# A Strassen scheme with seven block products for the first matrix of a second MLP, over pairs of token tiles

## The chip, the cores and the metric

One core of a Trainium2 chip. The time is the device time of one execution in microseconds; the kernel before takes 1283.23 us (median of 3 runs, 1282.59 to 1283.57). The engines are TensorE (PE, its weight loads PEld), VectorE (DVE), ScalarE (ACT), GpSimd (POOL), and SyncE (SP), whose queue issues nearly all DMAs.

## The reference

A linear attention over 8 batches of 8 heads, 576 tokens of 64 elements, then two MLPs over the 4608 tokens of width 512. In NumPy terms:

```python
x = attention(q, k, v).transpose(0, 2, 1, 3).reshape(4608, 512)
h = x @ w_in                                   # first network, 512 x 2048
x = (maximum(h, 0) + alpha * minimum(h, 0)) @ w_out
h = x @ w_in2                                  # second network, 512 x 1024
e = exp(h - max(h)); sm = e / (sum(e) + 1e-9)
solu = h * sm
ln = (solu - mean(solu)) / sqrt(var(solu) + 1e-6) * g_ln
out = ln @ w_out2                              # 1024 x 512
```

The change concerns `h = x @ w_in2` alone. All is float32.

## The kernel before

Every float32 operand of a large product is split in a high part (a rounded copy, written by ScalarE) and a low part (the operand less its high part, by VectorE or GpSimd), both in the type fp32r. A product is three matmuls: high by high, high by low weights, low by high weights. A matmul has a 128x128 stationary and a 128x512 moving operand.

The first network takes nine chunks of 512 tokens. For each it loops over 16 blocks `f` of the hidden width: `up(c, f)` (12 matmuls into `ps_h`), `prelu` on VectorE, `g_high` on ScalarE, `g_low` on GpSimd, and two blocks later `down(c, f)` (12 matmuls into `ps_y`). The attention of the next batch is worked in between. The result goes transposed to `y_scratch` in DRAM.

The second network takes 36 tiles of 128 tokens, written `tiles(m)` with `r` in 0 to 3. For each tile:

- SP loads `x2`; ScalarE makes `x2h` (line 769), GpSimd `x2l` (line 543).
- TensorE: `m1_product` (from line 1251), 24 matmuls with x stationary and `W2` moving, into two banks of `ps_m` or `ps_h`.
- VectorE: the negated maximum out of PSUM (line 1044). ScalarE: the exponential with its sum (line 734). VectorE: sum + eps, reciprocal, and `solu` = h * 1/sum * e, which reads h in PSUM (line 1057), its mean (line 1060). ScalarE: the squares (line 741). VectorE: variance (line 1066); GpSimd: to the power -1/2 (line 577); VectorE: `z` (line 1072) and its transpose in 32x32 blocks into `zb` (line 1078).
- SP stores `zb` to `z_scratch` (line 417) and loads it back with the blocks moved to their places as `zt`, in four DMAs (line 423). This completes the transpose. ScalarE makes `zh` (line 753), VectorE `zl` (line 1082).
- TensorE: `m2_product` (lines 1338 to 1340), 24 matmuls. ScalarE copies the result to `ost` (line 763), SP stores it.

The very last tile is transposed by TensorE instead (`z_transpose`, line 1325), since nothing is left to hide the way through DRAM.

All queues are written by hand, with counting semaphores. The order of the second network is a software pipeline: TensorE does `m1_product` of tile i + 1, then `m2_product` of tile i - 2. The first two `m1_product`s stand in the last chunk of the first network, between the last `down`s. The second network's weights are split during that chunk (lines 792 and 1035 for `w_in2`, 776 and 1024 for `w_out2`).

Of the kernel before, what the change touches and what calls it, by code (L numbers as in the profile page):

```python
# [26 lines left out]
def linear_attention_two_mlps(nc, q, k, v, w_in, w_out, alpha, w_in2, w_out2, g_ln, out):  # L27
# [24 lines left out]
    with ExitStack() as ctx:  # L52
# [7 lines left out]
        with ExitStack() as phase:  # L60
# [5 lines left out]
            qTh = sb("qTh", [P, 2, TOK], F32R)  # L66
            qTl = sb("qTl", [P, 2, TOK], F32R)
# [13 lines left out]
            kvh = sb("kvh", [P, KT, P], F32R)  # L81
            kvl = sb("kvl", [P, KT, P], F32R)
# [13 lines left out]
            mhalf = sb("mhalf", [P, 1])  # L96

# [5 lines left out]
        with ExitStack() as phase:  # L103
            W2 = sb("W2", [P, 2, KT, F2], F32R)
            WO2 = sb("WO2", [P, NF2, 2, DM], F32R)
            e2 = sb("e2", [P, 2, F2])
            solu = sb("solu", [P, 2, F2])
# [4 lines left out]
            ost = sb("ost", [P, 2, DM])  # L112
            st = sb("st", [P, 2, 10])
            zb = sb("zb", [P, F2])
            zt = sb("zt", [P, 2, F2])
# [6 lines left out]
        hbank = (ps_m, ps_h)  # L122
# [66 lines left out]
        x2_in = [sem(f"x2_in{i}") for i in range(4)]  # L189
        x2h_ok = sem("x2h_ok")  # L190
        x2l_ok = sem("x2l_ok")
        m1_done = sem("m1_done")
# [10 lines left out]
        zb_st = sem("zb_st")  # L203
        zb_ok = sem("zb_ok")
        zt_in = sem("zt_in")
# [8 lines left out]
        w2_at = {12: (0,), 13: (1, 2), 14: (3, 4), 15: (5, 6)}  # L214
        raw2 = (V[:, :, :, :].rearrange("p t h d -> p (t h d)")[:, 0:MAIN], A[:, 0:MAIN])

        x2 = (kmax[:, :].rearrange("p (a n) -> p a n", a=KT), x2b[:, :, :],
              V[:, :, :, :].rearrange("p t h d -> p (t h d)")[:, MAIN:MAIN + DM].rearrange("p (a n) -> p a n", a=KT),
              A[:, MAIN:MAIN + DM].rearrange("p (a n) -> p a n", a=KT))
        x2h, x2l = (t[:, :, :].rearrange("p s (a n) -> p s a n", a=KT) for t in (qTh, qTl))  # L220
# [8 lines left out]
        zb_out = zb[:, :].rearrange("p (j f a) -> p j f a", j=4, a=32)  # L229
# [4 lines left out]
        def z_source(r, by_pe):  # L234
            if by_pe:
                return z_blocks(ps_y[:, 0:2, :].rearrange("p a n -> p (a n)"))
# [61 lines left out]
        def _(sp):  # L298
# [93 lines left out]
            def load_x2(m, r, first=False):  # L392
                if first:
                    sp.wait_ge(y_st, 64 * (NC - 1))
                else:
                    sp.wait_ge(x2h_ok, 4 * m + r - 3)
                    sp.wait_ge(x2l_ok, 4 * m + r - 3)
                sp.dma_start(x2[r],
                             y_dram[m, :, :, r * P:(r + 1) * P].rearrange("a p n -> p a n")).then_inc(x2_in[r], 16)
# [13 lines left out]


            def store_z(m, r):
                sp.wait_ge(zb_ok, 4 * m + r + 1)
                sp.dma_start(z_dram[r % 2], zb[:, :]).then_inc(zb_st, 16)

            def load_z(m, r):

                sp.wait_ge(zb_st, 16 * (4 * m + r + 1))
                for j in range(4):
                    sp.dma_start(zt[32 * j:32 * (j + 1), r % 2, :].rearrange("b (i c) -> b i c", i=4),
                                 z_dram[r % 2].rearrange("(i b) (j c) -> j b i c", i=4, j=4)[j]).then_inc(zt_in, 16)

# [10 lines left out]
            for r in range(4):  # L436
                load_x2(0, r, first=True)
            sp.wait_ge(w2_hi, 2)
            sp.wait_ge(w2_lo, 2)
            sp.dma_start(raw2[0].rearrange("p (a n) -> p a n", a=half), w2o[:, 0:half, :]).then_inc(w2v_in, 16)  # L440
            sp.wait_ge(w2_hi, 4)
            sp.wait_ge(w2_lo, 4)
            sp.dma_start(raw2[1].rearrange("p (a n) -> p a n", a=half), w2o[:, half:NF2, :]).then_inc(w2a_in, 16)


            for r in range(4):
                if r >= 1:
                    load_z(0, r - 1)
                if r == 1:
                    store_y(LAST)  # L450
                load_x2(1, r)
                if r == 3:
                    store_out(0, 0)
                store_z(0, r)
            sp.wait_ge(y_st, 64 * NC)
            with sp.Fori(1, LAST) as m:
                for r in range(4):
                    if r == 0:
# [919 lines left out]
```

## Time and profile before

| | |
|---|---|
| median of 3 runs | 1283.23 us (1282.59 to 1283.57) |
| profiled execution | 1283.55 us, its span 1281.7 us |
| TensorE busy | 1269.4 us, 99% of the span |
| VectorE busy | 692.6 us, 54% |
| ScalarE busy | 387.3 us, 30% |
| GpSimd busy | 347.3 us, 27% |
| granted TensorE clock | 1.0 |

Busy is the time in which an engine has an instruction in execution. A matmul's row shows 0.39 us because the end of its way through the array is counted; matmuls overlap, and their pace is the distance from start to start. In the timeline the columns are start, duration, engine (SPq: a DMA issue on SP's queue), line, operation, output and inputs, and in square brackets the idle time ahead and what ended it.

### The profile page before, as it was taken

What the parts mean: (1) busy time and instruction counts of PE and PEld (TensorE: products, weight loads), DVE (VectorE), ACT (ScalarE), POOL (GpSimd) and SP (SyncE); (2) the same over time, 40 slices, a digit from 0 to 9 for tenths busy, and PEclk for the clock granted to TensorE, in tenths of its full rate; (3) what the DMA queues carried; (4) which work ended last, traced back from release to release, by engine and by line L of the source; (5) the groups of instructions that cost most, each with busy time, mean ns of one, the idle gap of its engine ahead of it and who ended that gap; (6) DMA issues with size and microseconds to landing.
All of it is one profiled execution on the core that took longest, in us unless ns stands there. A gap on an engine that the chain in (4) does not pass through costs nothing.

```text
span 1281.7 us, 16928 instructions
## 1 busy us (share of the span) xinstructions
PE 1269.4 (99%) x6277; PEld 1046.2 (82%) x6277; DVE 692.6 (54%) x965; ACT 387.3 (30%) x625; POOL 347.3 (27%) x289
## 2 busy tenths in 40 slices
PE   7999999999999999999999999999999999999998
PEld 6788888888888888888888888888888888888887
DVE  7865744644744644644644323346655555555553
ACT  4333212212222222222222212123544444444432
POOL 5333233233233234234234222222211111111110
PEclk9999999999999999999999999999999999999999
DMA  8543311311311311311310101210654444444432
GB/s 205 141 120 81 89 37 51 93 37 44 100 37 41 103 37 41 103 37 41 103 37 4 66 1 38 94 59 32 197 164 140 140 146 147 145 141 147 147 123 75
DMA packets 136017, 114.82 MB, mean 90 GB/s; under 512 B 56856, under 2 KB 117808, under 8 KB 135088
## 3 DMA queue, kind: packets, MB, share of 16 engines
q1 hardware_dynamic: 135936, 114.37, 30.2%
q8 instruction: 20, 0.33, 0.1%
q14 instruction: 13, 0.11, 0.0%
q10 hardware_dynamic: 48, 0.01, 0.0%
HBM read 76.03 MB, written 38.32 MB: 89 GB/s over the span
## 4 chain that ended last, share of the span: by engine, by line
PE 98%; DVE 1%; DMA 0%; issue 0%; POOL 0%; ACT 0%; DVEq 0%
PE ps_h L1202 10%; PE ps_y L1220 10%; PE ps_y L1218 10%; PE ps_y L1219 10%; PE ps_h L1204 10%; PE ps_h L1203 10%; PE ps_y L1339 5%; PE ps_y L1338 5%; PE ps_y L1340 5%; PE ps_h L1269 3%; PE ps_m L1273 3%; PE ps_m L1269 3%; PE ps_h L1273 3%; PE ps_m L1268 3%; PE ps_h L1268 3%; PE ps_m L1128 2%
## 5 line engine op out<-in xcount | busy, mean ns | idle before, releaser
L528 POOL TENSOR_TENSOR gl<-tg,gh 128x512 fp32r<-128x512 f32 x144 | 193.8, 1346 | 586.0 <-ACT gh L647 586.0
L647 ACT ACTIVATE gh<-tg 128x512 fp32r<-128x512 f32 x144 | 91.0, 632 | 598.4 <-PE ps_y L1220 432.3
L945 DVE TENSOR_SCALAR tg<-ps_h,acols 128x512 f32<-128x512 f32 x144 | 107.8, 748 | 242.2 <-PE ps_h L1204 240.7
L1202 PE MATMUL ps_h<-xh,W 128*128 128x512 f32 x576 | 227.5, 395 | 0.1
L1218 PE MATMUL ps_y<-gh,WO 128*128 128x512 f32 x576 | 225.3, 391 | 0.0
L1204 PE MATMUL ps_h<-xh,W 128*128 128x512 f32 x576 | 224.5, 390 | 0.0
L1220 PE MATMUL ps_y<-gh,WO 128*128 128x512 f32 x576 | 224.4, 390 | 0.0
L1203 PE MATMUL ps_h<-xl,W 128*128 128x512 f32 x576 | 224.3, 389 | 0.0
L1219 PE MATMUL ps_y<-gl,WO 128*128 128x512 f32 x576 | 224.2, 389 | 0.0
L1202 PEld LDWEIGHTS ps_h<-xh,W 128*128 128x128 f32 x576 | 108.1, 188 | 23.5 <-DVE W L936 0.5
L1204 PEld LDWEIGHTS ps_h<-xh,W 128*128 128x128 f32 x576 | 108.1, 188 | 23.0
L1220 PEld LDWEIGHTS ps_y<-gh,WO 128*128 128x128 f32 x576 | 108.1, 188 | 22.7
L1219 PEld LDWEIGHTS ps_y<-gl,WO 128*128 128x128 f32 x576 | 108.1, 188 | 22.1
L1218 PEld LDWEIGHTS ps_y<-gh,WO 128*128 128x128 f32 x576 | 108.2, 188 | 22.0
L1203 PEld LDWEIGHTS ps_h<-xl,W 128*128 128x128 f32 x576 | 108.2, 188 | 21.7
L1338 PE MATMUL ps_y<-WO,zh 128*128 128x512 f32 x288 | 112.1, 389 | 0.0
L1340 PE MATMUL ps_y<-WO,zl 128*128 128x512 f32 x288 | 112.0, 389 | 0.0
L1339 PE MATMUL ps_y<-WO,zh 128*128 128x512 f32 x288 | 112.0, 389 | 0.0
L948 DVE SCALAR_TENSOR_TENSOR tg<-ps_h,tg 128x512 f32<-128x512 f32 x144 | 99.5, 691 | 5.0
L1340 PEld LDWEIGHTS ps_y<-WO,zl 128*128 128x128 f32 x288 | 54.1, 188 | 11.3
L1338 PEld LDWEIGHTS ps_y<-WO,zh 128*128 128x128 f32 x288 | 54.0, 188 | 11.2
L1339 PEld LDWEIGHTS ps_y<-WO,zh 128*128 128x128 f32 x288 | 54.0, 187 | 11.1
(163 smaller groups left out, 1641.0 us busy)
## 6 DMA issues: line engine op xcount, KB each, us to landing
z_scratch<-zb SPq DMA_DIRECT2D x35, 512.0 KB, 2.6
zt<-z_scratch SPq DMA_DIRECT2D x140, 128.0 KB, 3.0
y_scratch<-stage SPq DMA_DIRECT2D x36, 256.0 KB, 3.1
A<-k_dram SPq DMA_DIRECT2D x16, 512.0 KB, 5.0
V<-v_dram SPq DMA_DIRECT2D x32, 256.0 KB, 4.7
out_dram<-ost SPq DMA_DIRECT2D x32, 256.0 KB, 2.3
A<-q_dram SPq DMA_DIRECT2D x14, 512.0 KB, 4.7
stage<-kx_scratch SPq DMA_DIRECT2D x6, 1024.0 KB, 4.6
```

The costliest lines, as they stand in the source:

```text
L528: nc.gpsimd.tensor_tensor(gl[:, f % 2, :], tg[:, f % 2, :], gh[:, f % 2, :].bitcast(F32), ALU.subtract).then_inc(gl_ok, 1)
L945: nc.vector.tensor_scalar(tg[:, f % 2, :], ps_h[:, f % 2, :], 0.0, slope[:, f:f + 1], ALU.min, ALU.mult).then_inc(t_ok, 1)
L948: nc.vector.scalar_tensor_tensor(tg[:, f % 2, :], ps_h[:, f % 2, :], 0.0, tg[:, f % 2, :], ALU.max, ALU.add).then_inc(g_ok, 1)
L1202: nc.tensor.matmul(o, W1[:, f, 0, a, :], xh[:, a, :], start=(a == 0), stop=False)
L1203: nc.tensor.matmul(o, W1[:, f, 0, a, :], xl[:, a, :], start=False, stop=False)
L1204: mm = nc.tensor.matmul(o, W1[:, f, 1, a, :], xh[:, a, :], start=False, stop=(a == KT - 1))
L1218: nc.tensor.matmul(o, WO[:, f, 0, cols], gh[:, f % 2, :], start=(f == 0), stop=False)
L1219: nc.tensor.matmul(o, WO[:, f, 0, cols], gl[:, f % 2, :], start=False, stop=False)
L1220: mm = nc.tensor.matmul(o, WO[:, f, 1, cols], gh[:, f % 2, :], start=False, stop=(f == NF - 1))
L1338: nc.tensor.matmul(o, zh[:, r % 2, f * P:(f + 1) * P], WO2[:, f, 0, :], start=(f == 0), stop=False)
L1339: nc.tensor.matmul(o, zh[:, r % 2, f * P:(f + 1) * P], WO2[:, f, 1, :], start=False, stop=False)
L1340: mm = nc.tensor.matmul(o, zl[:, r % 2, f * P:(f + 1) * P], WO2[:, f, 0, :], start=False, stop=(f == NF2 - 1))
```

## The change

Two tiles of 128 tokens are taken together, as a pair. x of the pair is cut in 2 x 2 blocks (two token tiles by two halves of the width 512), `w_in2` in 2 x 2 blocks of 256 x 512. Seven products of a block combination of x with one of w (Winograd's form of Strassen's scheme) give the four blocks of h:

- **Weights.** `w2_turn` on GpSimd forms the combinations in four subtractions in the last chunk; seven high parts (`w2_high`, ScalarE) and seven low parts (`w2_low`, VectorE) go to `W2c`.
- **x.** `x2_sums` on GpSimd makes four sums of 128x256 for each pair; then there are seven blocks of 128x256 to split, as one of 1024 and one of 768 elements: `x2_high` on ScalarE, `x2_low` on GpSimd (for the first two pairs VectorE). There is one buffer for these parts, free when all seven products of the pair before are done; `x2raw` has two.
- **Products.** `m1_pair` does seven groups of six matmuls in three banks (`ba`, `bb`, `bd`). The fourth adds onto the first's bank, the fifth onto the third's, the sixth onto the second's, the seventh again onto `bd`.
- **Sums out of PSUM.** ScalarE copies the first product to `p1` and the sum in `ba` to h's block 11. VectorE makes `q1`, `u1`, and the blocks c22, c12, c21 of h. h then stands in SBUF, in the tile `solu`, and the maximum, the exponential and the solu product read it there.
- **Order.** Each queue now goes pair by pair. TensorE: `m1_pair(i)`, then both `m2_product`s of pair i - 1. SP: both stores of z, then both loads. The last pair is transposed by TensorE, both tiles.
- **Start.** One `m1_pair` stands ahead of `down(14)` of the last chunk, in the place of the two single products.

TensorE's side:

```diff
+            def m1_pair(i, first=False):
+                pe.wait_ge(x2l_ok, 2 * i + 2)
+                if first:
+                    pe.wait_ge(w2_lo, 7)
+                    pe.wait_ge(g_ok, NF * LAST + 15)
+
+                def block(k, bank, more=False):
+                    a = LEFT[k] * 2 * P
+                    for j in range(2):
+                        hi, lo = (t[:, a + j * P:a + (j + 1) * P] for t in (x2h, x2l))
+                        nc.tensor.matmul(bank, hi, W2c[:, k, 0, j, :], start=(j == 0 and not more), stop=False,
+                                         skip_group_check=more)
+                        nc.tensor.matmul(bank, hi, W2c[:, k, 1, j, :], start=False, stop=False, skip_group_check=more)
+                        mm = nc.tensor.matmul(bank, lo, W2c[:, k, 0, j, :], start=False, stop=(j == 1), skip_group_check=more)
+                    mm.then_inc(prod, 1)
+
+                if not first:
+                    pe.wait_ge(c11_ok, i)
+                block(0, ba)
+                if not first:
+                    pe.wait_ge(c12_ok, i)
+                block(1, bb)
+                if not first:
+                    pe.wait_ge(c21_ok, i)
+                block(2, bd)
+                pe.wait_ge(p1_ok, i + 1)
+                block(3, ba, more=True)
+                pe.wait_ge(u1_ok, i + 1)
+                block(4, bd, more=True)
+                pe.wait_ge(q1_ok, i + 1)
+                block(5, bb, more=True)
+                pe.wait_ge(c22_ok, i + 1)
+                block(6, bd, more=True)
...
+            def pair(m, h, last=False):
+                i = 2 * m + h
+                m1_pair(i)
+                m2_product(i - 1, 0)
+                m2_product(i - 1, 1, last=(last and h == 1))
```

SP's order of a pair, its stores and loads of z:

```diff
+                for t in range(2):
+                    store_z(m, 2 * h + t)
+                if first and h == 0:
+                    sp.wait_ge(w2_lo, 7 + NF2)
+                for t in range(2):
+                    load_z(m, 2 * h + t)
```

ScalarE's:

```diff
+                p1_copy(i)
...
+                    zt_high(i - 1, 0)
+                c11_copy(i)
...
+                    zt_high(i - 1, 1)
+                if not (last and h == 1):
+                    x2_high(i + 1, 1 - h)
+                exp_tile(i, 0)
+                exp_tile(i, 1)
+                square_tile(i, 0)
+                square_tile(i, 1)
```

GpSimd's:

```diff
+            def x2_sums(i, h, m):
+                pool.wait_ge(x2_in[h], 32 * (m + 1))
+                a11, a12, a21, a22 = (x2raw[:, h, n * 2 * P:(n + 1) * 2 * P] for n in range(4))
+                s1, s2, s4 = (xsum[:, n * 2 * P:(n + 1) * 2 * P] for n in range(3))
+                if not (isinstance(i, int) and i == 0):
+                    pool.wait_ge(x2l_ok, 2 * i)
+                nc.gpsimd.tensor_tensor(s1, a21, a22, ALU.add).then_inc(xs_ok, 1)
...
+            def pair(m, h, first=False, last=False):
+                i = 2 * m + h
+                if not (last and h == 1):
+                    x2_sums(i + 1, 1 - h, m + h)
+                    if not (first and h == 0):
+                        x2_low(i + 1, 1 - h)
+                for t in range(2):
+                    power(m, 2 * h + t)
```

VectorE's order in the loop of the second network, before: two tiles (`ps_h` and `ps_m` hold h; `zl` belongs to a tile of two slots ago).

```order
L1082 TENSOR_TENSOR zl<-zt,zh 128x1024
...
L1057 SCALAR_TENSOR_TENSOR solu,st<-ps_m,st,e 128x1024
...
L1072 TENSOR_SCALAR z<-solu,st 128x1024
...
L1078 STREAM_TRANSPOSE zb<-z 128x1024
...
L1044 TENSOR_REDUCE st<-ps_h 128x1
...
L1082 TENSOR_TENSOR zl<-zt,zh 128x1024
```

And now, one pair. `kmt` is `q1`, `x2b` is `u1`, `kmax` is `p1`; the lines on `solu` with a sum are c22, c12 and c21; `A` holds what was loaded back as `zt`.

```order
L1147 TENSOR_TENSOR kmt<-ps_m,kmax 128x512
...
L1153 TENSOR_TENSOR x2b<-ps_h,kmax 128x512
...
L1162 TENSOR_TENSOR solu<-ps_h,kmt 128x512
...
L1219 TENSOR_TENSOR zl<-A,zh 128x1024
...
L1167 TENSOR_TENSOR solu<-ps_m,x2b 128x512
L1180 TENSOR_REDUCE st<-solu 128x1
...
L1171 TENSOR_TENSOR solu<-ps_h,kmax 128x512
L1180 TENSOR_REDUCE st<-solu 128x1
...
L1219 TENSOR_TENSOR zl<-A,zh 128x1024
...
L1189 SCALAR_TENSOR_TENSOR solu,st<-solu,st,e 128x1024
```

The first `zl` has moved between the sums of the pair's products, and both `zl` stand ahead of the solu products of both tiles; two normalisations with their transposes follow.

SP's queue in the same loop, before, for one tile and the start of the next:

```order
L423 DMA zt<-z_scratch 32x4x256 x4
...
L398 DMA kmax<-y_scratch 128x4x128
...
L410 DMA out_dram<-ost 128x512
...
L417 DMA z_scratch<-zb 128x1024
...
L423 DMA zt<-z_scratch 32x4x256 x4
...
L398 DMA x2b<-y_scratch 128x4x128
```

And now, for one pair (`tg` holds the output, `V` the transposed z):

```order
L435 DMA out_dram<-tg 128x512
...
L422 DMA x2raw<-y_scratch 128x4x128
...
L422 DMA x2raw<-y_scratch 128x4x128
...
L435 DMA out_dram<-tg 128x512
...
L440 DMA z_scratch<-V 128x1024
...
L440 DMA z_scratch<-V 128x1024
...
L446 DMA A<-z_scratch 32x4x256 x8
```

The load of a tile stood ahead of the next tile's store; now both stores stand ahead of both loads.

## Rows read from the trace of the kernel before

**Rows 1.** The page: span, and busy time of each engine.
```profile
span 1281.7 us, 16928 instructions
...
PE 1269.4 (99%) x6277; PEld 1046.2 (82%) x6277; DVE 692.6 (54%) x965; ACT 387.3 (30%) x625; POOL 347.3 (27%) x289
```

**Rows 2.** Timeline, second network: first matmuls of an `m2_product` and the next group.
```profile
1004.68 0.39 PE L1338 MATMUL ps_y<-WO,zh 128*128 128x512 f32 x1
...
1010.12 0.39 PE L1268 MATMUL ps_h<-W,qTh 128*128 128x512 f32 x1
```

**Rows 3.** Timeline of VectorE, one tile in a dense stretch.
```profile
903.94 1.19 DVE L1044 TENSOR_REDUCE st<-ps_m 128x1 f32<-128x1024 f32 x1
905.05 1.20 DVE L1082 TENSOR_TENSOR zl<-zt,zh 128x1024 fp32r<-128x1024 f32 x1
906.40 0.15 DVE L1053 TENSOR_SCALAR st<-st 128x1 f32<-128x1 f32 x1
...
908.11 0.15 DVE L1060 TENSOR_SCALAR st<-st 128x1 f32<-128x1 f32 x1
909.57 0.15 DVE L1066 TENSOR_SCALAR st<-st 128x1 f32<-128x1 f32 x1 [1.31 <-ACT junk L741]
...
912.41 1.19 DVE L1044 TENSOR_REDUCE st<-ps_h 128x1 f32<-128x1024 f32 x1
```

**Rows 4.** Groups by line (count | busy us, mean ns | idle before).
```profile
L932 DVE TENSOR_TENSOR xl<-ps_m,xh 128x512 fp32r<-128x512 f32 x28 | 19.4, 692 | 45.9 <-ACT xh L636 45.9
...
L753 ACT ACTIVATE zh<-zt 128x1024 fp32r<-128x1024 f32 x35 | 37.0, 1056 | 7.8 <-DMA zt<-z_scratch 7.8
...
L636 ACT ACTIVATE xh<-ps_m 128x512 fp32r<-128x512 f32 x28 | 16.8, 598 | 30.7 <-PE ps_m L1179 30.7
```

**Rows 5.** Timelines of GpSimd and VectorE, operations that meet, and two that don't.
```profile
864.20 1.29 POOL L528 TENSOR_TENSOR gl<-tg,gh 128x512 fp32r<-128x512 f32 x1 [4.14 <-ACT gh L647]
...
864.78 1.26 DVE L1024 SCALAR_TENSOR_TENSOR WO<-V,acols,WO 128x512 fp32r<-128x512 f32 x1 [2.25 <-ACT WO L776]
...
888.30 0.75 DVE L1024 SCALAR_TENSOR_TENSOR WO<-A,acols,WO 128x512 fp32r<-128x512 f32 x1 [1.88 <-ACT WO L776]
...
483.90 0.17 DVE L919 TENSOR_SCALAR qe<-qs 128x16 f32<-128x16 f32 x1
...
486.00 2.90 POOL L518 TENSOR_TENSOR V<-A,qr 64x512 f32<-64x512 f32 x2
...
486.91 2.02 DVE L919 TENSOR_SCALAR qe<-qs 128x16 f32<-128x16 f32 x1
...
1007.76 1.28 DVE L1057 SCALAR_TENSOR_TENSOR solu<-ps_m,st,e 128x1024 f32<-128x1024 f32 x1
...
1007.94 1.29 POOL L543 TENSOR_TENSOR qTl<-V,qTh 128x512 fp32r<-128x512 f32 x1 [7.49 <-ACT qTh L769]
```

**Rows 6.** Timelines of SP's queue and ScalarE: store, loads, and the `zh` that waited.
```profile
906.96 1.74 SPq L423 DMA_DIRECT2D zt<-z_scratch  x4
...
912.51 0.34 SPq L417 DMA_DIRECT2D z_scratch<-zb  x1
915.15 1.74 SPq L423 DMA_DIRECT2D zt<-z_scratch  x4
...
912.59 1.06 ACT L753 ACTIVATE zh<-zt 128x1024 fp32r<-128x1024 f32 x1 [3.05 <-DMA zt<-z_scratch]
...
919.62 1.06 ACT L753 ACTIVATE zh<-zt 128x1024 fp32r<-128x1024 f32 x1 [0.98 <-DMA zt<-z_scratch]
```

**Rows 7.** Timeline of TensorE: the first matmul behind the last `up`.
```profile
876.84 0.39 PE L1218 MATMUL ps_y<-gh,WO 128*128 128x512 f32 x1
```

**Rows 8.** Timelines of TensorE and ScalarE at the end: transposes, last copy.
```profile
1265.80 1.03 PE L1325 MATMUL ps_y<-ident,z 128*128 128x128 f32 x8
...
1277.77 0.60 ACT L763 ACTIVATE ost<-ps_y 128x512 f32<-128x512 f32 x1 [4.84 <-PE ps_y L1340]
```

**Rows 9.** Windows: busy us of PE, PEld, DVE, ACT, POOL; granted clock, DMA share, GB/s.
```profile
40.00:44.00 4.00, 2.54 (x14) 1.87 (x13) 3.86 (x5) 0.00 (x0) 0.00 (x0) 1.00 0.91 187
```

More of the change, by code:

```diff
@@ L468, in _ @@
[L468 to L478 removed]
+                for h in range(2):
+                    pair(m, h)
+            for h in range(2):
+                pair(LAST, h, last=True)
@@ new lines, in _ @@
+            for h in range(2):
+                pair(0, h, first=True)
+            with act.Fori(1, LAST) as m:
+                for h in range(2):
+                    pair(m, h)
+            for h in range(2):
+                pair(LAST, h, last=True)
+            zt_high(2 * LAST + 1, 0, by_pe=True)
+            out_copy(2 * LAST, 1, last=True)
+            zt_high(2 * LAST + 1, 1, by_pe=True)
+            out_copy(2 * LAST + 1, 0, last=True)
+            out_copy(2 * LAST + 1, 1, last=True)
@@ L1085, in tiles @@
-            def tiles(m, first=False, last=False):
-                for r in range(4):
-                    softmax_tile(m, r, first=first)
-                    norm_tile(m, r, by_pe=(last and r == 3))
-            tiles(0, first=True)
-            with dve.Fori(1, LAST) as m:
-                tiles(m)
-            tiles(LAST, last=True)
-            zt_low(LAST, 2)
-            zt_low(LAST, 3, by_pe=True)
+                        dve.wait_ge(zb_st[t], 16 * i)
+                    nc.vector.transpose(zb_out(t), zb_in).then_inc(zb_ok, 1)
@@ L1098, in _ @@
+            for h in range(2):
+                pair(0, h, first=True)
+            with dve.Fori(1, LAST) as m:
+                for h in range(2):
+                    pair(m, h)
+            for h in range(2):
+                pair(LAST, h, last=True)
+            for t in range(2):
+                zt_low(2 * LAST + 1, t, by_pe=True)
         @block.tensor
@@ L1304, in chunk @@
                 for what in tail:
-                    if last and what == "y" and piece % KT == 0:
-                        m1_product(0, piece // KT, first=True)
+                    if last and what == "y" and piece == 0:
+                        m1_pair(0, first=True)
                     if what == "y":
@@ L1343, in tiles @@
-            def tiles(m, first=False, last=False):
-                for r in range(4):
-                    if not (first and r == 0 or last and r == 3):
-                        m1_product(m + (r + 1) // 4, (r + 1) % 4, first=(first and r < 3))
-                    if r >= 2:
-                        m2_product(m, r - 2, first=first)
-                    elif not first:
-                        m2_product(m - 1, r + 2)
-            tiles(0, first=True)
-            with pe.Fori(1, LAST) as m:
-                tiles(m)
@@ new lines, in pair @@
+            def pair(m, h, last=False):
+                i = 2 * m + h
+                m1_pair(i)
+                m2_product(i - 1, 0)
+                m2_product(i - 1, 1, last=(last and h == 1))
+            pair(0, 1)
+            with pe.Fori(1, LAST) as m:
+                for h in range(2):
+                    pair(m, h)
+            for h in range(2):
+                pair(LAST, h, last=True)
+            z_transpose(2 * LAST + 1, 1)
+            for t in range(2):
+                m2_product(2 * LAST + 1, t)
```

566 lines of the change are left out of this document (327 added, 239 removed).

## The prediction

> **What bounds the kernel now.** I read the page first, then the waits, then the order of time of one steady stretch of the second network. TensorE is busy for 1269.4 of 1281.7 us [rows 1], and the granted clock is the full one everywhere. In the second network the matmuls follow each other without a gap: the 24 matmuls of one `m2_product` start at 1004.68 and the next group starts at 1010.12, so 24 matmuls take 5.44 us and one takes 0.2267 us [rows 2]. What matters for the change is how much time the other engines have left. Before, a pair of token tiles costs TensorE 96 matmuls, 21.76 us. VectorE needs for one tile, start to start, 1.11 (maximum), 1.18 (`zl` subtraction), 1.86 (the small operations and the solu product, 906.40 to the end of the operation at 908.11), and 2.84 (variance to the end of the transpose, 909.57 to 912.41) [rows 3]: 7.0 us of a 10.88 us slot. So the chain of one tile ends well inside its slot and its way through DRAM and back is hidden.
>
> **What the change removes.** Seven products of six matmuls take the place of two groups of 24, 42 for 48. That is 6 x 18 pairs = 108 matmuls, 108 x 0.2267 = 24.5 us of TensorE. A pair now costs TensorE 90 matmuls, 20.4 us. If TensorE stayed the bound, this would be the gain, less the start below.
>
> **What it adds for a pair.** VectorE gets five 128x512 sums with one operand in PSUM. The nearest row, a subtraction of that shape, takes 0.69 us, and dense ones step by 0.61 to 0.65 [rows 4]; I take 0.63 each. ScalarE gets two copies of 0.6. GpSimd gets four 128x256 sums, and its low parts grow from two of 512 to 1024 + 768 elements. A 128x512 subtraction of GpSimd takes 1.29 [rows 5], so the four are about 0.65 each and the two 2.5 and 1.9; these are estimates by size. The maximum now reads SBUF, as does the solu product; I leave their times as they are.
>
> **The new loop.** The order text shows the point on which I rest. `zl` of the pair before, first tile, stands *between* c22 and c12 on VectorE; everything of the present pair's softmax stands behind it. And SP now stores both transposed tiles before it loads the first one back. So a closed chain goes once around per pair: transpose of the second tile, store, load of the first, `zh`, `zl`, the rest of VectorE's work of the pair, transpose of the second tile. Let E be the end of that transpose. Steps after E:
>
> - SP issues the store of the second tile (0.35), then the load of the first, whose store is long done. From the first load issue to the `zh` that waited for it: 919.62 - 915.15 = 4.47, and 912.59 - 906.96 = 5.63 [rows 6]. Here the store moves ahead of it, which is for it a little more; I take 4.65, near the shorter one, whose pattern is the ordinary one, and keep 5.63 for the range. `zh` starts at E + 5.0 and takes 1.06 [rows 4]: `zl` can start at E + 6.1.
> - `zl` 1.18, c12 0.63, maximum 1.11, c21 0.63, maximum 1.11: E + 10.75. The PSUM sums' products are ready before that.
> - `zl` of the second tile 1.18, two solu steps of 1.86, two normalisations of 2.84, and 0.1 to the end of the last: E + 21.4.
>
> So even if nothing else goes wrong the loop takes 21.4, more than TensorE's 20.4.
>
> **The waits between VectorE and GpSimd.** Rows 5 show that the two exclude each other for some shapes. An SBUF-only product on VectorE takes 0.75 alone and 1.26 when GpSimd's subtraction began before it, and it ends 0.55 after GpSimd does (865.49 and 866.04). A 128x16 tensor_scalar, 0.17 elsewhere, takes 2.02 and ends with GpSimd's pair of multiplications. But the solu product out of PSUM takes 1.28 with GpSimd's subtraction beside it, as always. Before, the VectorE operation that meets GpSimd in the steady part of the second network is this one, so nothing is lost. After, three meet it and don't:
>
> - ScalarE reaches the pair's first x high part after `zh` of the second tile. The second load waits for its store (2.64, 912.51 to 915.15 [rows 6]), so `zh` runs from E + 7.4 to 8.45, the x copy to 9.5, and GpSimd's 1024-element low part from 9.55 to 12.05. `zl` of the second tile wants to start at 10.75. It ends about 1.1 after GpSimd, at 13.15: 1.2 late.
> - GpSimd's second part then goes from 13.15 to 15.0. The first solu product, now SBUF by SBUF, wants to start at 13.5, and its step ends at 16.45: 1.4 late.
> - GpSimd's first sum of the next pair starts with the end of the second power, just ahead of the second `z` (SBUF to SBUF tensor_scalar): 0.5 late.
>
> The loop is 21.4 + 1.2 + 1.4 + 0.5 = **24.6 us** rounded up. Bounds: 21.4 if these three cost nothing, and 24.6 + 1.0 for the longer landing + 0.9 for further sums of GpSimd that get ahead of VectorE, 26.5. I take 24.6, since rows 5 are of the same operations. TensorE then waits 4.2 us in each pair, split over the fourth and fifth product and the two `m2_product`s.
>
> **The two ends.** Last chunk of the first network: TensorE ends its last `up` at 876.84 [rows 7] and `down(13)` at 879.56. Before, the first x high part was made chunks of time ahead; now it waits for that `up` (one buffer), 1.05 + 0.83 on ScalarE and 0.9 for the last low part: product 1 starts at 880.3. Four small conversions of `w_out2` ahead of the sums cost some 0.6; seventh product at 890.5, two `down`s to 895.9. VectorE, with eight such conversions and the second x pair among the first pair's work, gets to E(0) at about 907.8: from 891.0, c21 0.6, x low parts 2.3, maximum 1.1, four conversions 2.7 at some 0.67 each, then 2 x 1.86 + 2 x 2.84 + 0.7 for GpSimd's first sum and the end of the last step. The second pair's products wait for it meanwhile. From E(0) there are sixteen loops to E(16). Then the last pair: its normalised tiles go by TensorE. `zl` ready at +7.3; with no x work left there is no lock and `z` is ready at +17.3; 8 transposes 0.8 [rows 8], the second half of the product to +21.0, the second transposes +21.8, two products to +32.7, and from the last copy to the span's end 1281.7 - 1277.77 = 3.9 [rows 8]: E(16) + 36.8.
>
> **Sum.** 907.8 + 16 x 24.6 + 36.8 = 1338.2 of span. The profiled execution took 1283.55 for a span of 1281.7, 1.85 more, and lies 0.3 over the median 1283.23. So **1340 us**. The other way round: 1283.6 - 24.5 + 16 x 4.2 of waits + 11 at the start + 2 at the end + 0.8 of transposes = 1340.
>
> **The clock.** TensorE will stand still in stretches of 1 to 2.5 us. In the stretch 40 to 44 us it was busy 2.54 of 4 and the granted clock stayed at 1.00, the 2.4 GHz level [rows 9]. So I cost this at nothing. The Trainium skill (TensorE: Matmul & The Clock Gate, on the two states of the clock) says that an array that has been idle long enough falls to 1.2 GHz, which speaks against every change that turns a dense kernel into one with waits. By it the matmuls of a pair could take twice their time.
>
> **Rivals.** (1) *The lock costs little*, because the transfers or ScalarE shift GpSimd's work to a place where VectorE reads PSUM. For it: GpSimd has only some 8 us of work in 24. Against: its low parts come right behind `zh` of the second tile. The loop is 21.4 to 23.4, 1290 to 1321 us. (2) *Faster: the loop never binds.* If the tile is back early, `zl` and c12 follow their products at once, and the three GpSimd waits fall into time in which VectorE waits anyway for TensorE; the loop is then TensorE's 20.4, 1340 - 16 x 4.2 = 1273 us. The point of decision is a loop of (1281.7 - 36.8 - 907.8) / 16 = 21.1 us: below, faster than before. Against it: VectorE's own work after the landing has no gap in which to hide anything, and it would need 3.5 us off the chain. (3) *Slower landing and more locks*, a loop above 26: over 1363 us. (4) *The clock falls*: with a pair's 90 matmuls wholly at 1.2 GHz the loop would be 40.8, near 1600 us; rows 9 speak against it. That it doesn't do what it says I can exclude: the order shows 42 matmuls a pair.
>
> **How the numbers follow.** Forecast, a loop of 23.4 to 26 us (1321 to 1363): 0.60. Rival 1: 0.20. Rival 2: 0.10. Rival 3: 0.08. Rival 4: 0.02. The range from 1290 to 1365 takes in the forecast and rival 1 and leaves out 0.2. A measurement of this kernel can tell some 0.2% from no change. Faster by more than that is rival 2, 0.10; within 0.2% is a loop within 0.15 of 21.1, 0.02; slower is the rest, 0.88.
>
> **What would show it.** In the changed profile: TensorE's busy share near 93%; `m2_product` of the first tile waiting for `zl`; ScalarE's `zh` waiting for the DMA some 2 us or more in each pair; `zl` of the second tile and the first solu product on VectorE well above 1.2 and 1.28 us; transposes 24 to 25 us apart from pair to pair. If `zl` and solu have their old durations, rival 1 holds; if TensorE waits for nothing between pairs, the loop was wrong.

## The result and the profile after

| | before | after |
|---|---|---|
| median of 4 runs | 1283.40 us (1282.59 to 1284.28) | 1336.49 us (1335.22 to 1337.18) |
| profiled execution, its span | 1283.55, 1281.7 us | 1337.0, 1335.2 us |
| granted clock, mean over the span | 1.00 | 0.985 |

After against before is a ratio of 1.0413, with an interval of 1.0396 to 1.0429: 4.1% slower. The forecast was 1340 us.

The page of the changed kernel: the span, the busy times of the engines, TensorE and the clock in 40 slices of 33.4 us, and one of the costliest groups.

```profile
span 1335.2 us, 17241 instructions
PE 1271.2 (95%) x6177; PEld 1035.9 (78%) x6177; DVE 783.2 (59%) x1061; ACT 420.2 (31%) x664; POOL 449.9 (34%) x361
...
PE   7999999999999999999999999998888898988997
...
PEclk9999999999999999999999999998999999899999
...
L826 ACT ACTIVATE zh<-A 128x1024 fp32r<-128x1024 f32 x34 | 36.0, 1059 | 146.1 <-DMA A<-z_scratch 146.1
```

Against [rows 1] all engines but TensorE got more work, as expected, and TensorE has lost most of its 9s in the last third of the span, the second network. The curious number is TensorE's busy time: it issues 108 matmuls of the products fewer, 24.5 us (the count falls by 100, since the end has eight short transposes more), and was busy 1271.2 us against 1269.4. So what it saved in matmuls it spent again, some 26 us; the part on the clock below comes back to that. ScalarE stood still 146.1 us ahead of its 34 `zh` conversions, each time until the loads of the transposed tile had landed.

The waits between 930 and 1270 us, some fourteen pairs (engine, line, what released it: us in total, times, longest):

```profile
ACT zh L826 <- DMA A<-z_scratch: 120.5, 28, 9.0
...
DVE zl L1219 <- ACT zh L826: 38.0, 14, 3.3
PEld ps_y L1521 <- issue: 36.2, 14, 3.2
PE ps_y L1521 <- DVE zl L1219: 30.5, 15, 2.8
```

Read from below: TensorE's `m2_product` waits for `zl`, `zl` on VectorE waits for `zh`, `zh` on ScalarE waits for the loads. That is the chain on which the forecast rested. Its other half is on VectorE itself. Here is one pair of it, from the second transpose (the E of the prediction, 1077.31 + 1.25 = 1078.56) to the next one. Left out are the products' sums, the maxima and the operations on columns. Columns: start, duration, engine, line, operation; in brackets the idle time before it and what ended that.

```profile
1077.31 1.25 DVE L1213 STREAM_TRANSPOSE V<-z 128x1024 f32<-128x1024 f32 x1
...
1085.45 1.23 DVE L1219 TENSOR_TENSOR zl<-A,zh 128x1024 fp32r<-128x1024 f32 x1 [2.80 <-ACT zh L826]
...
1090.36 1.65 DVE L1219 TENSOR_TENSOR zl<-A,zh 128x1024 fp32r<-128x1024 f32 x1
...
1092.31 2.49 DVE L1189 SCALAR_TENSOR_TENSOR solu<-solu,st,e 128x1024 f32<-128x1024 f32 x1
...
1095.32 1.29 DVE L1189 SCALAR_TENSOR_TENSOR solu<-solu,st,e 128x1024 f32<-128x1024 f32 x1
...
1097.53 0.82 DVE L1207 TENSOR_SCALAR z<-solu,st 128x1024 f32<-128x1024 f32 x1 [0.66 <-POOL st L629]
...
1100.42 1.22 DVE L1207 TENSOR_SCALAR z<-solu,st 128x1024 f32<-128x1024 f32 x1 [0.67 <-POOL st L629]
1101.68 1.25 DVE L1213 STREAM_TRANSPOSE V<-z 128x1024 f32<-128x1024 f32 x1
```

From E to the `zl` of the first tile is 1085.45 - 1078.56 = 6.9 us. From there to the end of the next second transpose, 1102.93, is 17.5 us. Together 24.4: the loop, once around. Two equal operations stand in this stretch with two durations, `zl` with 1.23 and 1.65 and the solu product with 2.49 and 1.29. GpSimd's row beside them says why:

```profile
1088.54 2.39 POOL L577 TENSOR_TENSOR xl<-x2raw,xh 128x1024 fp32r<-128x1024 f32 x1 [9.25 <-ACT xh L846]
1090.87 2.84 POOL L577 TENSOR_TENSOR xl<-xsum,xh 128x768 fp32r<-128x768 f32 x1
...
1100.35 0.74 POOL L566 TENSOR_TENSOR xsum<-x2raw 128x256 f32<-128x256 f32 x1
```

The second `zl` was to start when the maximum was through, 1090.4, and GpSimd's first low part ended at 1090.93; the first solu product was to start at 1092.31 and the second low part ended at 1093.71, and VectorE's operation ends 1.09 after that (1094.80). The second `z` meets the start of GpSimd's sum. These are the three meetings of the forecast.

SP's queue and ScalarE over the same turn show the trip:

```profile
1075.39 3.52 SPq L440 DMA_DIRECT2D z_scratch<-V  x2
1079.05 4.21 SPq L446 DMA_DIRECT2D A<-z_scratch  x8
```

```profile
1084.36 1.06 ACT L826 ACTIVATE zh<-A 128x1024 fp32r<-128x1024 f32 x1 [7.34 <-DMA A<-z_scratch]
...
1086.45 1.06 ACT L826 ACTIVATE zh<-A 128x1024 fp32r<-128x1024 f32 x1 [0.56 <-DMA A<-z_scratch]
```

SP issues both stores (the 3.52 us of their row go from the first issue to the end of the second), and only then the first of the eight loads, at 1079.05, 0.5 after E. `zh` starts 5.31 later.

### The profile page after: what moved, and what is told of

Its sections match the earlier page's. It is cut to its first block and busy times, and to the rows that moved or that the text cites. A ratio compares the mean times of both kernels' runs of the same rounds, so it can differ in the third digit from the quotient of the medians.

```text
span 1335.2 us, 17241 instructions
## 1 busy us (share of the span) xinstructions
PE 1271.2 (95%) x6177; PEld 1035.9 (78%) x6177; DVE 783.2 (59%) x1061; ACT 420.2 (31%) x664; POOL 449.9 (34%) x361
## 5 line engine op out<-in xcount | busy, mean ns | idle before, releaser
L1521 PE MATMUL ps_y<-WO,zh 128*128 128x512 f32 x288 | 119.8, 416 | 35.0 <-DVE zl L1219 34.9
L1385 PEld LDWEIGHTS ps_y<-gh,WO 128*128 128x128 f32 x576 | 108.2, 188 | 22.5
L1522 PE MATMUL ps_y<-WO,zh 128*128 128x512 f32 x288 | 117.4, 408 | 0.0
L1523 PE MATMUL ps_y<-WO,zl 128*128 128x512 f32 x288 | 117.3, 407 | 0.0
L1521 PEld LDWEIGHTS ps_y<-WO,zh 128*128 128x128 f32 x288 | 57.0, 198 | 55.2 <-issue 36.2
L577 POOL TENSOR_TENSOR xl<-x2raw,xh 128x1024 fp32r<-128x1024 f32 x16 | 38.4, 2403 | 148.1 <-ACT xh L846 148.1
L826 ACT ACTIVATE zh<-A 128x1024 fp32r<-128x1024 f32 x34 | 36.0, 1059 | 146.1 <-DMA A<-z_scratch 146.1
```

The lines of the kernel that those rows point to most:

```text
L1385: mm = nc.tensor.matmul(o, WO[:, f, 1, cols], gh[:, f % 2, :], start=False, stop=(f == NF - 1))
L1521: nc.tensor.matmul(o, zh[:, t, f * P:(f + 1) * P], WO2[:, f, 0, :], start=(f == 0), stop=False)
L1522: nc.tensor.matmul(o, zh[:, t, f * P:(f + 1) * P], WO2[:, f, 1, :], start=False, stop=False)
L1523: mm = nc.tensor.matmul(o, zl[:, t, f * P:(f + 1) * P], WO2[:, f, 0, :], start=False, stop=(f == NF2 - 1))
```

## The experiments

My theory: the span is a start, sixteen turns of the closed loop and an end, and the loop consists of the trip through DRAM, VectorE's work behind it, and what the meetings with GpSimd add. The main rival: TensorE is slow for another reason, the clock that is lower around its waits, or its own start; then taking parts of the loop away brings little.

**Trip away, meetings away, both away.** Three kernels, which share a chip and a run of before of 1282.59 us. The first keeps the tile in its buffer and sends it nowhere, so its output lacks the second half of the transpose, and the loop's DMAs of z are gone with it:

```diff
-                for t in range(2):
-                    store_z(m, 2 * h + t)
...
-                for t in range(2):
-                    load_z(m, 2 * h + t)
...
-            return zt[:, r % 2, :]...
+            return zb[:, r % 2, :]...
...
-                    act.wait_ge(zt_in[t], 64 * (i + 1))
+                    act.wait_ge(zb_ok, 2 * i + t + 1)
...
-                    dve.wait_ge(zb_st[t], 16 * i)
+                    dve.wait_ge(zl_ok, 2 * i)
```

> Edit: the way of z through DRAM is left out. No store and no load of z; ScalarE's zh and VectorE's zl read the block-transposed zb of the pair before directly, as soon as the transpose is done. The output then lacks the second half of the transpose; every engine keeps its instructions. Theory 1 (the closed loop: trip, zl, rest of VectorE's pair, transpose): the trip's 5.8 us go and VectorE's first zl follows c22 at once; the chain behind it is 21.3 us with the waits against GpSimd, so the loop falls from 24.3 to about 21.3 and the span from 1335 to about 1287. Theory 2 (VectorE's and GpSimd's own work binds, the trip is beside the point): span stays above 1325. Theory 3 (TensorE's clock dips of this trace bind): loop above 23, span above 1315.

The second shortens GpSimd's low parts of the x tiles to 128 columns each and leaves the low parts of the other columns stale:

```diff
-    nc.gpsimd.tensor_tensor(x2l[:, lo:hi], src, x2h[:, lo:hi].bitcast(F32),
+    nc.gpsimd.tensor_tensor(x2l[:, lo:lo + P], src[:, 0:P], x2h[:, lo:lo + P].bitcast(F32),
```

> Edit: GpSimd's two low parts of x are made over the first 128 columns each in place of 1024 and 768 (the low parts of the other columns are left stale from the second pair on), so GpSimd holds nothing while VectorE does zl of the second tile and the first solu product. Theory 1: zl falls from 1.8 to 1.2 us and the first solu product from 2.5 to 1.3, the loop from 24.3 to about 22.5, the span to about 1306. Theory 2 (the exclusion is hidden by other waits, the trip alone sets the loop): span within 5 us of 1335.

The third has both edits.

> Edit: both of the former two together (no way through DRAM, low parts of 128 columns). Theory 1: VectorE's chain is then under 20.4 us, so TensorE is the bound, with a loop of 20.4 us; the span is about 1270, and TensorE waits for nothing from the third pair on. This would show the full 24.5 us of the seven products, less the start. Theory 2: if something not in my sum binds (ScalarE, SP, the clock), the loop stays above 21 and the span above 1280.

Measured, one execution each, with the loop read from the first and the last second transpose of VectorE (the columns after the count: shortest, median, longest in ns, and the first and last start):

```profile
L1213 DVE STREAM_TRANSPOSE V<-z x34: 1244/1245/1247, 903.5 to 1295.8; 128x1024 f32<-128x1024 f32 x34
```

```profile
L1207 DVE STREAM_TRANSPOSE V<-z x34: 1244/1245/1247, 902.7 to 1245.5; 128x1024 f32<-128x1024 f32 x34
```

```profile
L1213 DVE STREAM_TRANSPOSE V<-z x34: 1245/1246/1246, 902.8 to 1266.6; 128x1024 f32<-128x1024 f32 x34
```

```profile
L1207 DVE STREAM_TRANSPOSE V<-z x34: 1245/1246/1247, 902.5 to 1232.4; 128x1024 f32<-128x1024 f32 x34
```

These are the changed kernel, without the trip, with short low parts, and with both. The first start is that of the first tile of the first pair; the second tile's is 3.2 later in all four (906.69 in the changed kernel). So the loop is (last - first - 3.2) / 16:

| kernel | time, us | its span, us | loop, us | TensorE's waits from 930 us to the last pair |
|---|---|---|---|---|
| changed | 1337.0 | 1335.2 | 24.3 | 37.2 us in 14 pairs |
| without the trip | 1282.96 | 1281.2 | 21.2 | 6.1 us |
| short low parts | 1307.5 | 1305.7 | 22.5 | 21.7 us |
| both | 1271.41 | 1269.6 | 20.4 | none |

The whole loss lies in these two. With both taken away the loop is TensorE's own 20.4 us, and the time is that of rival 2 in the forecast, 1273. And the kernel without the trip, with a loop of 21.2, takes 1282.96 us against 1282.59 of before beside it, close to the point of decision that the forecast put at 21.1. That it fits so well is in part luck: from E of the last pair to the end this kernel needs 34.5 us and the changed kernel 38.2, and with the latter's end the point would lie at 21.0. The expected spans of the kernel with short low parts and of the one with both were met within 0.4 us (1305.7 for 1306, 1269.6 for 1270). The one without the trip had the expected loop, but its span, 1281.2, is 6 us under the expected 1287, mostly since I had not counted on the shorter end.

In the kernel without the trip the meetings with GpSimd that the short low parts take away are still there, but cost less, 21.2 - 20.4 = 0.8 us a turn. Its c22 sum with VectorE's wait for TensorE, and its first solu product, as long as ever:

```profile
1060.26 0.69 DVE L1156 TENSOR_TENSOR solu<-ps_h,kmt 128x512 f32<-128x512 f32 x1 [1.84 <-PE ps_h L1426]
...
1067.82 2.49 DVE L1183 SCALAR_TENSOR_TENSOR solu<-solu,st,e 128x1024 f32<-128x1024 f32 x1
```

And with both edits the first sums and the same product:

```profile
1051.80 0.69 DVE L1147 TENSOR_TENSOR x2b<-ps_h,kmax 128x512 f32<-128x512 f32 x1 [0.51 <-PE ps_h L1426]
...
1054.62 0.69 DVE L1156 TENSOR_TENSOR solu<-ps_h,kmt 128x512 f32<-128x512 f32 x1 [2.12 <-PE ps_h L1426]
...
1061.65 1.28 DVE L1183 SCALAR_TENSOR_TENSOR solu<-solu,st,e 128x1024 f32<-128x1024 f32 x1
```

The product is back to 1.28 us, and VectorE waits for TensorE twice in a turn, 2.6 us. Where the trip is gone, GpSimd first uses up this time, and only the rest of what it takes lengthens the turn. So the two edits' own gains, 3.1 and 1.8 us a turn, add up to more than the 3.9 from 24.3 down to TensorE's 20.4: below that the loop can't go.

**The loads of the first tile ahead of the store of the second.** The forecast laid part of the trip to SP's order. Here SP takes the tiles one by one:

```diff
                 for t in range(2):
                     store_z(m, 2 * h + t)
-                if first and h == 0:
-                    sp.wait_ge(w2_lo, 7 + NF2)
-                for t in range(2):
+                    if first and h == 0 and t == 0:
+                        sp.wait_ge(w2_lo, 7 + NF2)
                     load_z(m, 2 * h + t)
```

> Edit: SP stores and loads the first tile, then stores and loads the second (two stores then two loads in the changed kernel). Theory 1: zh of the first tile starts at E + 3.9 in place of + 5.8. But the rest of the chain then meets GpSimd's low parts fully (both solu products, as zh of the second tile and so the x parts come no earlier), so of the 1.9 us only 0.4 to 1.8 come back: loop 22.5 to 23.9, span 1307 to 1329. Theory 2 (the pair order of the stores doesn't matter, landing is set by the DMA engines): span within 4 us of 1335.

Measured 1329.67 us in one execution, 7.3 less than the changed kernel in its profiled execution. The span, 1327.8, and the loop, 23.9, are at the upper end of what was expected: nearly a miss. SP's queue and ScalarE in one pair, E at 1074.6:

```profile
1074.05 1.74 SPq L446 DMA_DIRECT2D A<-z_scratch  x4
1075.91 0.36 SPq L440 DMA_DIRECT2D z_scratch<-V  x1
1079.35 1.73 SPq L446 DMA_DIRECT2D A<-z_scratch  x4
```

```profile
1078.43 1.06 ACT L825 ACTIVATE zh<-A 128x1024 fp32r<-128x1024 f32 x1 [7.22 <-DMA A<-z_scratch]
1083.64 1.06 ACT L825 ACTIVATE zh<-A 128x1024 fp32r<-128x1024 f32 x1 [3.67 <-DMA A<-z_scratch]
```

The first tile is back 3.8 us after E and not 5.8, so `zl` of the first tile hardly holds TensorE up any more (4.5 us of waits from 930 to 1230, where the changed kernel has 26.5). But the second store is issued behind four loads, 1.3 us after its tile was ready, and the second tile's loads could be issued only when it was through, 3.44 us later (1075.91 to 1079.35). So the second tile is back at E + 9.0, where it was 7.9, and its `zl` comes late in its turn. TensorE's waits, from 930 to 1250, have gone to the fifth product, which needs the sum `u1` that VectorE makes only after the transposes of the pair before. VectorE itself now waits for something new, ScalarE's exponential, which stands behind the late `zh` and the x copies in ScalarE's order, 1.6 us a turn:

```profile
PE ps_h L1428 <- DVE x2b L1152: 26.6, 14, 2.5
...
DVE st L1184 <- ACT e L805: 20.6, 13, 1.6
```

So most of the 2.0 us that the first tile won is lost again behind the second. In this order of the two, one tile is late as well, only another one.

**The loop opened.** If the loop is too long because one turn has to hold the trip and VectorE's whole work, the cure is to give it two turns: TensorE multiplies with the transposed tiles of the pair before the last.

```diff
             def pair(m, h):
                 i = 2 * m + h
                 m1_pair(i)
-                m2_product(i - 1, 0)
-                m2_product(i - 1, 1, last=(last and h == 1))
+                m2_product(i - 2, 0)
+                m2_product(i - 2, 1)
```

With it ScalarE makes `zh` of the first tile between the two squares of its pair and that of the second at the head of the next one, and VectorE makes `zl` ahead of each tile's `z` and last transpose. GpSimd gets a wait, so that its sums start only when VectorE has gone over to operations that read PSUM:

```diff
                 if not (last and h == 1):
+                    pool.wait_ge(q1_ok, i + 1)
                     x2_sums(i + 1, 1 - h, m + h)
```

> Edit, all parts of the computation kept: the second products of a pair go one pair later (TensorE: m1_pair(i), then m2_product of pair i - 2), so zh and zl of pair i - 1 may be made anywhere in pair i; VectorE does zl of the first tile while it waits for the first power and zl of the second between z and the last transpose; ScalarE's second zh moves to the next pair's start; GpSimd's sums of x wait until q1 is made, when VectorE reads PSUM. Theory 1 (closed loop through DRAM plus exclusion): the trip leaves the loop, which is then VectorE's work alone, at or under TensorE's 20.4 us. It costs a longer start, since the first three m1_pairs follow each other and wait for VectorE (some 12 us more), so the span is about 1280, near the kernel before. Theory 2 (exclusion alone already holds the loop at 21.3, as in the run without the trip): span about 1295.

Measured 1279.7 us in one execution, with a span of 1277.9. The expected 1280 held. Between 930 and 1268 us TensorE waits for nothing any more; what is left are waits in the first pairs, where the second network has nothing yet to multiply. A second version moves the P1 copy and the first two sums of pair 1 ahead, between pair 0's operations:

```diff
                 solu_tile(i, 0)
+                if start:
+                    q1_sum(1)
+                    u1_sum(1)
                 solu_tile(i, 1)
```

> Edit: the former, and in the first pair p1, q1 and u1 of the second pair are made before the first pair's softmax is through (ScalarE's copy behind the exponentials, VectorE's sums behind the first solu product), so that TensorE gets to the sixth product of the second pair without waiting. Theory 1: the start's wait falls by some 2.5 us, c22 of the second pair follows the first pair's last transpose at once; span about 1278, a loop of 20.4 to 20.5. Theory 2 (the start is bound elsewhere): no difference from the former.

Measured 1278.50 us as the median of 6 runs (1277.44 to 1279.79) beside 9 of before (1282.65 to 1283.71): a ratio of 0.9963, with an interval of 0.9950 to 0.9975. **This version is faster than both kernels**, by 0.4% than before and 58 us than the changed one. Its windows (busy us of PE, PEld, DVE, ACT, POOL with the number of instructions; granted clock, DMA share, GB/s):

```profile
876.20:931.05 54.85, 40.89 (x156) 31.61 (x155) 44.44 (x66) 27.61 (x43) 19.32 (x19) 0.84 0.40 128
931.05:1268.00 336.95, 336.95 (x1496) 279.08 (x1495) 260.60 (x397) 170.35 (x256) 149.66 (x118) 1.00 0.48 143
```

From 931 to 1268 us TensorE doesn't stand still at all, at the full clock, with the trip and with GpSimd's full low parts. What is left of the price is the first row: 13.96 us of 54.85 idle, with a granted clock of 0.84 in the mean. These are the start's waits:

```profile
PE ps_m L1453 <- POOL xl L577: 6.4, 1, 6.4
PE ps_h L1453 <- DVE solu L1171: 4.6, 1, 4.6
PE ps_h L1453 <- DVE x2b L1162: 2.2, 1, 2.2
```

So of the 24.5 us of matmuls saved, 4.35 arrive in the time. Of the other 20.1, 13.96 are this idle time, and some 5.5 the lower clock in the same window, by an estimate: its 156 matmuls took 40.9 us and would take 35.4 at 0.2267 each.

**GpSimd's wait taken out again**, to see whether the meetings matter when the loop is open:

```diff
-                    pool.wait_ge(q1_ok, i + 1)
                     x2_sums(i + 1, 1 - h, m + h)
```

> Edit: the former, but GpSimd's sums of x stand where the changed kernel has them, straight behind the second power, so they meet z, zl and the transposes' neighbours on VectorE. Theory 1: 0.4 to 1.1 us of exclusion come back in each pair. VectorE has no slack left, so the loop goes to 20.8 to 21.4 and the span to 1284 to 1294. Theory 2: VectorE has slack; span within 2 us of the former.

Measured 1293.55 us in one execution, 14.3 more than the profiled execution of the version with the wait, for one wait less. The two traces side by side, VectorE at the same place of a pair, first with the wait and then without:

```profile
1066.98 0.81 DVE L1219 TENSOR_SCALAR z<-solu,st 128x1024 f32<-128x1024 f32 x1
1067.71 1.22 DVE L1232 TENSOR_TENSOR zl<-A,zh 128x1024 fp32r<-128x1024 f32 x1
```

```profile
1073.79 1.29 DVE L1218 TENSOR_SCALAR z<-solu,st 128x1024 f32<-128x1024 f32 x1
1075.00 1.75 DVE L1231 TENSOR_TENSOR zl<-A,zh 128x1024 fp32r<-128x1024 f32 x1
```

GpSimd's sums, each of 0.74 us alone, cost VectorE 0.48 and 0.53 us, 1.0 a pair; the two that ran into them took 1.18 and 1.72 themselves. TensorE waits for `x2b` in each pair (8.8 us in 14 between 931 and 1268). From the first to the last of 28 transposes it is now 280.5 us, and was 268.3: 0.9 in each of the 13 turns between them. So the opened loop, too, has a closed chain with next to nothing to spare: `u1` on VectorE, TensorE's fifth product, c22 on VectorE, which waits for it 1.94 us with the wait of GpSimd and 1.84 without, and the rest of VectorE's pair to the next `u1`. A meeting in it is paid nearly in full.

**The start filled.** The last version puts the first `m2_product` between the first layers of pairs 1 and 2, where TensorE was waiting, and moves its `zh` and `zl` forward to the first exponential and the first solu product of pair 1:

```diff
             m1_pair(1)
+            m2_product(0, 0)
             for h in range(2):
                 pair(1, h)
```

> Edit, all parts of the computation kept: the kernel of the run before with the early sums kept (e6), and the first m2_product (pair 0, first tile) put between the m1_pairs 1 and 2, where TensorE waits 6.5 us for GpSimd's low parts; its zh and zl are moved ahead of the second exponential and the second solu product of pair 1. Theory 1 (the loop is TensorE's, only the start still waits): the 5.44 us of the product fill that wait and the wait of 2.2 for u1 behind it, VectorE's work is only moved; span 1277 - 5 = 1272, faster than the kernel before by 0.7%. Theory 2 (VectorE's chain at the start holds everything behind it): span 1275 to 1278.

This was a miss: 1282.79 us, median of 10 runs, ratio to before 1.0001 (0.9992 to 1.0011), where I expected 1272. Two rows show where it went, `zl` on VectorE and the first matmul of the product:

```profile
916.28 2.63 DVE L1234 TENSOR_TENSOR zl<-A,zh 128x1024 fp32r<-128x1024 f32 x1
```

```profile
918.97 0.79 PE L1549 MATMUL ps_y<-WO,zh 128*128 128x512 f32 x1 [7.53 <-DVE zl L1234]
```

TensorE stood still 7.5 us for this `zl`. It fell on GpSimd's low part and took 2.63 us in place of 1.22, but that is only 1.4 of the 7.5. The rest is its place: behind the exponential and the first solu product of pair 1, which began at 914.88, when TensorE had been waiting since 911.4. Then, with only one `m2_product` left between the first layers of pairs 2 and 3, TensorE ran ahead of VectorE again, and waited 2.9 us for `x2b` at 952. TensorE's waits from 850 to 1000 us are 17.2 us in all (7.5 + 4.6 + 2.9 + 1.0 + 0.6 + 0.6), against 13.8 (6.4 + 4.6 + 2.2 + 0.6) in the version without the fill. I had counted the filler as 5.44 us of work and its place as free; but the work ahead of it had to be ready there, and wasn't. Whether another place for it does better was not tried.

## Why the forecast was right, and where it was not

**The sign, the mechanism and the sum were right, partly by two errors that cancel.** The sum against the trace:

| term | forecast | measured |
|---|---|---|
| product 1 starts | 880.3 | 880.6 |
| E(0) | 907.8 | 907.9 |
| E to `zh` of the first tile | 5.0 | 5.8, in the mean of 16 turns 5.6 |
| `zl` of the second tile late | 1.2 | 0.4, in the mean of 14 pairs 0.6 |
| first solu product late | 1.4 | 1.2 |
| second `z` late | 0.5 | 0.4 |
| loop | 24.6 | 24.3 |
| E(16) to the end | 36.8 | 38.2 |
| span | 1338.2 | 1335.2 |

With the measured terms the sum closes: 907.9 + 16 x 24.32 + 38.15 = 1335.2. Where a single turn is shown it is the one from 1078.56 us. The good E(0) is luck in part: c21 of the first pair began at 891.9 and not 891.0, and the work behind it took 0.8 us less than the forecast's sum.

**What the saved matmuls bring.** The forecast said that TensorE would need 20.4 us for a pair. The kernel with both edits has exactly this loop.

**The landing was undersized.** I took 4.65 us from the first load issue to `zh`, near the shorter of the two cases of [rows 6]. It took 5.31 in the turn shown and 4.85 to 5.50 in the sixteen turns, 5.15 in the mean, between the two. The choice by "whose pattern is the ordinary one" was the step that failed. After the change the loads follow right behind a second store of 512 KB, with four more loads behind them. In the kernel that stores and loads tile by tile, with neither, it is 4.10 to 4.63 us for every tile from 930 to 1250 us. Which of the two makes the difference, the store or the other loads, no run separates. With 0.14 more until SP's first load issue this is the 0.8 by which the trip was too short in the turn shown, and 0.6 in the mean.

**The meetings were oversized**, by 1.1 us in the turn shown and 0.9 in the mean, and mostly in one of three. The second `zl` was to come 1.2 late, since GpSimd's low part was to run from E + 9.55 to 12.05. But the longer landing moved `zl` of the first tile back by 0.8 and that of the second by 1.05, while ScalarE's x copy moved back by only 0.4: in the turn shown, GpSimd's low part ran from E + 9.98 to 12.37, and `zl` came to it at E + 11.8. So the two errors are linked: what the trip took longer, the meeting took less. The price of the meetings comes out the same in two ways. By durations it is 0.4 + 1.2 + 0.4 = 2.0 us in the turn shown. And from the `zl` of the first tile to the end of the next second transpose it is 17.5 us there, and 15.85 with short low parts (1049.67 to 1065.52 in that trace): 1.6 for the two meetings at `zl` and solu, while the third, at `z`, is in both.

**TensorE's waits.** Forecast 4.2 us a pair, from (24.6 - 20.4). In the trace they are 37.2 us in 14 pairs, 2.7 a pair (30.5 for `zl`, 6.7 for `x2b`). The rest of the 3.9 between the loop and 20.4 isn't idle time but matmuls at the lower clock. The forecast of a busy share of 93% was a miss for the same reason; it is 95%.

**The clock.** The forecast gave it nothing, by a single row of the start [rows 9], and this was wrong as a statement and right for the sum. Behind the wait of the turn shown the matmuls go at half their pace for some 4 us:

```profile
1086.80 0.49 PE L1521 MATMUL ps_y<-WO,zh 128*128 128x512 f32 x1 [2.27 <-DVE zl L1219]
...
1087.88 0.63 PE L1521 MATMUL ps_y<-WO,zh 128*128 128x512 f32 x1
1088.30 0.63 PE L1522 MATMUL ps_y<-WO,zh 128*128 128x512 f32 x1
...
1091.25 0.39 PE L1521 MATMUL ps_y<-WO,zh 128*128 128x512 f32 x1
```

Their rows show 0.63 us, and they start 0.42 us apart, not 0.227. But TensorE is not what the loop waits for: between `zl` of the first tile and the next second transpose VectorE waits for no product, and TensorE has 3.9 us to spare in each turn, out of which the slow matmuls take 1.2 in the mean (3.9 less 2.7 of waits), some 20 us in sixteen turns. The rest of the 26 us was not taken apart. So I read the clock's fall as free here, for the loop; at the start and the end it may have a part. The kernels without waits speak for the waits as its cause: with both edits, and in the version that beats before, the granted clock from 930 to 1230 us is 1.00 and no matmul group is above 391 ns in the mean, where the clock is 0.97 and `m2_product`'s groups are 409 to 417 in the changed kernel. The length of the waits counts: without the trip TensorE waits 0.4 us in each pair, and the clock is 1.00 too. Rival 4, all matmuls of a pair at half the clock, didn't come about; a mild form of it did. By the Trainium skill (TensorE: Matmul & The Clock Gate) an array that has been idle falls to the lower clock: the trace agrees, with a wait for `zl` of 2.0 us in the mean in every turn, more clearly than I had granted.

**The end.** 1.35 us more than forecast; I have not taken it apart. The forecast's own terms, 32.7 + 3.9, give 36.6 and not 36.8. Another reading was off too: between the starts of `zl` and the next operation [rows 3] shows 1.35 us and not 1.18; in the kernel with both edits it is 1.13.

**The rivals.** Rival 1 said that the lock costs little. With 2.0 us a turn against the 3.1 forecast it has a part of the truth, but the measured loop of 24.3 lies outside its 21.4 to 23.4, and would even with the shorter landing (23.7). Rival 2's time, 1273, is what the kernel with trip and meetings taken away shows (1271.4): the arithmetic of this case was right, and its condition not met. Rival 3, a loop above 26, didn't come about.

## What to carry to other kernels

When matmuls are saved in a kernel that is bound by TensorE, first write down the longest closed chain that goes once around per iteration (work of the other engines, plus a trip through DRAM, plus the wait for whoever comes before it in order), and compare it with TensorE's new, shorter time: before the change there was a reserve, and the change both shortens the time and adds to the chain. If the chain is the longer one, it can be cheaper to let the consumer lag by one more iteration (1336.5 to 1278.5 us here) than to shorten its parts; here taking away either the trip or GpSimd's low parts alone didn't get below the kernel before. The lag has its price in the prologue, and there work that is moved into a gap helps only if what it needs is ready by then.

## What the runs showed of the hardware that was not expected

- A trip of two 512 KB tiles through DRAM: from the issue of the first load, behind two stores, until its consumer starts, 4.85 to 5.50 us. With four loads ahead of a store, that store took 3.44 us from issue to the release of the load behind it, against 2.64 in [rows 6].
- With waits of at most 2.8 us that come back in every turn of 24 us the granted clock fell in parts: 0.86 in a window of the loop with 2.26 us of idle time, and 1.00 in the next, which has no wait; around the wait of 4.87 us at the start of the second network it was 0.62 (windows of 12.3 us; columns as above). Waits of at most 0.4 us a turn, in the kernel without the trip, left it at 1.00:

```profile
900.00:912.30 12.30, 6.87 (x17) 4.66 (x16) 7.77 (x15) 4.91 (x9) 4.25 (x6) 0.62 0.37 127
936.80:949.10 12.30, 10.04 (x37) 7.82 (x36) 10.02 (x14) 7.33 (x10) 5.17 (x2) 0.86 0.42 103
949.10:961.40 12.30, 12.30 (x56) 10.18 (x55) 7.65 (x12) 3.50 (x7) 4.28 (x6) 1.00 0.48 159
```

- Small sums on GpSimd are not free beside VectorE: four of them, of 0.74 us each alone, made the `z` and the `zl` that ran beside them 0.48 and 0.53 us longer. Beside VectorE operations that read PSUM they cost nothing: all four took 0.74 us there, and `u1` and c22 on VectorE 0.67 and 0.69. The Trainium skill (SBUF — State Buffer, on who interferes with whom) says that a VectorE instruction with two inputs in SBUF contends with a GpSimd instruction that reads SBUF, and that one with at most one such input doesn't, outside VectorE's two-port modes: the `zl` rows with 1.22 and 1.75 us agree. `z` has one input in SBUF and was lengthened as well; whether it ran in such a mode no run shows.
